# Attention with hashed buckets and two feed-forward layers: q and k arrive feature first, GpSimd splits them, and TensorE no longer transposes them

## What is computed

```
q_bits = (q @ proj > 0);  k_bits = (k @ proj > 0)      # proj is 64 x 6
mask   = (bucket(q_bits)[:, None] == bucket(k_bits)[None, :])
scores = where(mask, 0.125 * q @ k.T, -1e9)
x      = softmax(scores) @ v                            # 16 heads, 768 x 64 each
h = x @ w1_in;  g = where(h > 0, h, exp(min(h, 0)) - 1);  x = g @ w1_out
h = x @ w2_in;  g = s * max(h, 0)**2 + b;                 x = g @ w2_out
```

## Time and profile before

| | |
|---|---|
| median of 3 runs | 829.45 us (828.56 to 829.95) |
| span of the profiled execution, first to last instruction | 824.9 us |
| outside the span, by the runs | 3.7 to 5.1 us |
| TensorE busy | 809.9 us, 98% |
| VectorE, ScalarE, GpSimd busy | 445.3, 364.7, 181.0 us |
| attention | about 0 to 290 us, 17.5 us a head |
| feed-forward | about 290 to 825 us |

### The profile page before, as it was taken

The page is one execution under the profiler, slowest core; times in us unless marked ns, Lnnn a source line. Parts: engine busy times, 40 slices in busy tenths (PEclk is TensorE's granted clock), DMA queues, the critical chain, the costliest instruction groups (busy, mean ns, idle before and its releaser), DMA issues.

```text
span 824.9 us, 12868 instructions
## 1 busy us (share of the span) xinstructions
PE 809.9 (98%) x4252; PEld 697.6 (85%) x4252; DVE 445.3 (54%) x780; ACT 364.7 (44%) x735; POOL 181.0 (22%) x160
## 2 busy tenths in 40 slices
PE   7999999999999999999999999999999999999998
PEld 6799999999999977888888888887888888888886
DVE  6888888888888839533333343335223432243323
ACT  4888888888888831123221222213221222222221
POOL 3243332334322209400000036663000000000000
PEclk9999999999999999999999999999999999999999
DMA  3423243232323013200000012330000100010001
GB/s 97 120 59 94 76 103 91 57 92 74 87 68 88 1 52 125 80 1 0 1 1 1 0 33 94 102 102 26 1 1 0 51 0 0 0 51 0 0 0 51
DMA packets 34359, 38.70 MB, mean 47 GB/s; under 512 B 3168, under 2 KB 25824, under 8 KB 34336
## 3 DMA queue, kind: packets, MB, share of 16 engines
q1 hardware_dynamic: 33744, 38.22, 16.0%
q10 hardware_dynamic: 592, 0.17, 0.1%
HBM read 26.38 MB, written 3.15 MB: 36 GB/s over the span
## 4 chain that ended last, share of the span: by engine, by line
PE 94%; DVE 3%; DMA 1%; ACT 1%; issue 0%; SPq 0%; ACTq 0%; DVEq 0%
PE acc L521 31%; PE h_ps L503 31%; PE pt_ps L466 8%; PE s_ps L457 4%; PE pv_ps L479 4%; PE pv_ps L480 4%; PE s_ps L458 4%; PE prep_ps L434 2%; PE pv_ps L489 2%; PE prep_ps L429 2%; PE prep_ps L439 1%; DVE g_lo L879 1%; PE prep_ps L446 1%; DVE pt_lo L759 1%; DMA qt<-qt 0%
## 5 line engine op out<-in xcount | busy, mean ns | idle before, releaser
L721 ACT ACTIVATE r_sb<-h_ps 128x512 f32<-128x512 f32 x96 | 57.4, 598 | 359.4 <-PE h_ps L503 359.4
L873 DVE TENSOR_SCALAR g_sb<-e_sb,sb_scale 128x512 f32<-128x512 f32 x48 | 26.2, 546 | 158.1 <-ACT e_sb L724 158.1
L759 DVE TENSOR_TENSOR pt_lo<-pt_ps,pt_hi 128x384 fp32r<-128x384 f32 x192 | 103.4, 552 | 13.2 <-ACT pt_hi L627 11.3
L871 DVE SCALAR_TENSOR_TENSOR g_sb<-e_sb,h_ps 128x512 f32<-128x512 f32 x48 | 32.9, 686 | 132.2 <-ACT e_sb L724 132.2
L627 ACT ACTIVATE pt_hi<-pt_ps 128x384 fp32r<-128x384 f32 x192 | 93.4, 494 | 24.5 <-PE pt_ps L466 23.7
L752 DVE TENSOR_REDUCE row_min<-s_ps 128x1 f32<-128x768 f32 x96 | 91.4, 953 | 21.0 <-PE s_ps L458 20.5
L466 PE MATMUL pt_ps<-cst,probs 128*128 128x128 f32 x576 | 95.8, 277 | 1.5 <-DVE pt_lo L759 1.5
L647 ACT ACTIVATE probs<-s_ps,row_min 128x768 f32<-128x768 f32 x96 | 86.7, 904 | 0.9
L879 DVE TENSOR_TENSOR g_lo<-g_sb,g_hi 128x512 fp32r<-128x512 f32 x96 | 80.5, 838 | 3.3
L466 PEld LDWEIGHTS pt_ps<-cst,probs 128*128 128x128 f32 x576 | 68.6, 140 | 12.4 <-issue 6.0
L503 PE MATMUL h_ps<-xt_hi,wa_hi 128*128 (+1 forms) x192 | 75.1, 391 | 0.4 <-DVEq L856 0.4
(11 more groups left out here) (118 smaller groups left out, 1613.2 us busy)
## 6 DMA issues: line engine op xcount, KB each, us to landing
w_raw<-w_in_dram SPq DMA_DIRECT2D x32, 256.0 KB, 2.8
w_raw<-w_out_dram SPq DMA_DIRECT2D x32, 256.0 KB, 2.9
kt<-kt SPq DMA_DIRECT2D x30, 192.0 KB, 2.9
raw_q<-q_dram SPq DMA_DIRECT2D x16, 192.0 KB, 2.4
raw_k<-k_dram SPq DMA_DIRECT2D x16, 192.0 KB, 2.5
raw_v<-v_dram SPq DMA_DIRECT2D x16, 192.0 KB, 2.4
out_dram<-o_sb SPq DMA_DIRECT2D x12, 256.0 KB, 2.1
qt<-qt SPq DMA_DIRECT2D x15, 192.0 KB, 3.7
```

The source lines that it names most:

```text
L759: tt(pt_lo[(k // HT) % 2][where], pt_ps[n][:, 0:HALF].rearrange("p (t c) -> p t c", t=HT), pt_hi[(k // HT) % 2][where].bitcast(F32), ALU.s ...
```

## The change

The host now lays q and k out as `qk[head, feature, {q, k}, token]` and v so that a tile holds consecutive tokens. Every row of SBUF is a feature: rows 0 to 63 and rows 64 to 127 both get all 64 features, of q and of k. The cycles QA to KB are gone with `q_nat`, `k_nat`, `ident_r` and ScalarE's four copies; four cycles stay, in the same units and places. The projections take three matmuls a half (`kt1` holds k hi in both halves, `kt2` k lo over q hi, `qt1` q hi over q lo). GpSimd scales q, rounds and subtracts; SyncE copies q hi twice and k hi no longer.

```diff
-PLAN = ((QA, None, QB), (KA, None, KB), (ZA, None, ZB), (EA, None, None), (EB, None, None), (None, None, None))
+PLAN = ((ZA, None, ZB), (EA, None, None), (EB, None, None), (None, None, None), (None, None, None), (None, None, None))
...
             def load_qk(head):
-                wait(sp, k_split, head)
-                sp.dma_start(raw_q[:].rearrange("p t d -> p (t d)"), row(q_d, head)).then_inc(qk_in, 16)
-                sp.dma_start(raw_k[:].rearrange("p t d -> p (t d)"), row(k_d, head)).then_inc(qk_in, 16)
+                sp.wait_ge(q_split, head)
+                sp.wait_ge(k_split, head)
+                for rows in (slice(0, DH), slice(DH, P)):
+                    sp.dma_start(raw_qk(rows), row(qk, head)).then_inc(qk_in, 16)
+            def load_first():
+                for n, raw, landed in ((0, raw_q, q0_in), (1, raw_k, k0_in)):
+                    for rows in (slice(DH, P), slice(0, DH)):
+                        sp.dma_start(raw[rows, :], qk[0, :, n, :]).then_inc(landed, 16)
...
             def copy_hi(head, par):
-                sp.wait_ge(prep_act, len(BY_ACT) * head + KB + 1)
-                k_hi_rows = kt2[par][DH:P, :].bitcast(F32)
-                sp.dma_start(kt1[par][0:DH, :].bitcast(F32), k_hi_rows).then_inc(hi_copied, 16)
-                sp.dma_start(kt1[par][DH:P, :].bitcast(F32), k_hi_rows).then_inc(hi_copied, 16)
-                sp.dma_start(qt2[par][0:DH, :].bitcast(F32), qt1[par][0:DH, :].bitcast(F32)).then_inc(hi_copied, 16)
+                sp.wait_ge(q_hi, head + 1)
+                q_hi_rows = kt2[par][DH:P, :].bitcast(F32)
+                sp.dma_start(qt1[par][0:DH, :].bitcast(F32), q_hi_rows).then_inc(hi_copied, 16)
+                sp.dma_start(qt2[par][0:DH, :].bitcast(F32), q_hi_rows).then_inc(hi_copied, 16)
+            def step(head, par, v=True, qk=True, copy=True):
+                if v:
+                    load_v(head + 2)
+                if copy:
+                    copy_hi(head + 2, par)
+                if qk:
+                    load_qk(head + 3)
+            def pair(i):
+                step(2 * i, 0)
+                step(2 * i + 1, 1)
+                load_w(0, i, 0, i)
+            load_first()
+            load_v(0)
+            sp.wait_ge(hi_copied, 32)
             load_qk(1)
+            copy_hi(1, 1)
+            load_v(1)
             load_qk(2)
...
             def split_qk(head, par):
...
+                low = slice(DH, P)
+                pool.wait_ge(qk_in, 32 * head)
+                wait(pool, scores_done, TILES * (head - 1))
                 pool.nop(nofuse=True)
+                nc.gpsimd.tensor_scalar(raw_q[:], raw_q[:], -SCALE, 1.0, ALU.mult, ALU.mult).then_inc(q_scaled, 1)
+                nc.gpsimd.tensor_copy(kt1[par][:], raw_k[:]).then_inc(k_hi, 1)
+                pool.wait_ge(q_scaled, head)
+                pool.wait_ge(k_hi, head + 1)
                 pool.nop(nofuse=True)
+                nc.gpsimd.tensor_copy(kt2[par][low, :], raw_q[low, :]).then_inc(q_hi, 1)
+                nc.gpsimd.tensor_tensor(kt2[par][0:DH, :], raw_k[0:DH, :], kt1[par][0:DH, :].bitcast(F32),
+                                        ALU.subtract).then_inc(k_split, 1)
                 pool.wait_ge(q_hi, head + 1)
+                nc.gpsimd.tensor_tensor(qt1[par][low, :], raw_q[low, :], kt2[par][low, :].bitcast(F32),
+                                        ALU.subtract).then_inc(q_split, 1)
+                pool.wait_ge(k_split, head + 1)
+                pool.wait_ge(q_split, head + 1)
...
             def pair(i, more=True):
                 split_v(2 * i + 1, 1)
-                split_qk(2 * i + 3, 1)
-                split_v(2 * i + 2, 0)
                 if more:
-                    split_qk(2 * i + 4, 0)
+                    split_qk(2 * i + 2, 0)
+                    split_v(2 * i + 2, 0)
+                    split_qk(2 * i + 3, 1)
                 split_w(at(wa_hi, i), at(wa_lo, i), i, 0, i + 1)
...
             def prepare(head, par, cycle, bank=prep_ps[:]):
+                if cycle == ZA:
+                    pe.wait_ge(k_split, head + 1)
+                    pe.wait_ge(q_split, head + 1)
+                    pe.wait_ge(hi_copied, 32 * head + 32)
+                if cycle <= ZB:
+                    for j, x in enumerate((kt1, kt2, qt1)):
+                        last = mm(dst, plane(n, j), x[par][:, cols], start=n == 0 and j == 0, stop=n == 1 and j == 2)
...
+            act.wait_ge(q0_in, 32)
+            copy(kt2[0][DH:P, :], raw_q[DH:P, :], -SCALE).then_inc(q_hi, 1)
+            copy(qt1[0][0:DH, :], raw_q[0:DH, :], -SCALE).then_inc(hi_copied, 16)
+            copy(qt2[0][0:DH, :], raw_q[0:DH, :], -SCALE).then_inc(hi_copied, 16)
...
+            nc.vector.scalar_tensor_tensor(qt1[0][low, :], raw_q[low, :], -SCALE, kt2[0][low, :].bitcast(F32),
+                                           ALU.mult, ALU.subtract).then_inc(q_split, 1)
+            dve.wait_ge(k_hi, 1)
+            tt(kt2[0][top, :], raw_k[top, :], kt1[0][top, :].bitcast(F32), ALU.subtract).then_inc(k_split, 1)
```

More of the change, by code:

```diff
@@ L40 @@
 GROUPS = UNITS // HT
-CYCLES = 8
+CYCLES = 4
 TOKENS = BATCH * SEQ
@@ L70, in uses @@
 def uses(k):
[L72 to L74 removed]
+    t, off = k % TILES, k // TILES + 1
+    got = [None if c is None else (off, c) for c in PLAN[t]]
     if k in X_UNIT:
@@ L423, in prepare @@
                 dst = bank[:, 0:HALF]
-                if cycle <= KB:
-                    src, ready = (q_nat, q_split) if cycle <= QB else (k_nat, k_split)
-                    if n == 0:
-                        pe.wait_ge(ready, head + 1)
-                    for r in range(HT):
-                        last = nc.tensor.transpose(bank[:, r * P:(r + 1) * P].bitcast(F32R),
-                                                   src[par][:, n * HT + r, :], ident_r[:])
-                elif cycle <= ZB:
-                    for j, x in enumerate((qt1, qt1, kt2, kt2)):
-                        last = mm(dst, planes[:, n, j, :], x[par][:, cols], start=n == 0 and j == 0, stop=n == 1 and j == 3)
+                if cycle == ZA:
[5 more added lines that the diff above has]
+                        last = mm(dst, plane(n, j), x[par][:, cols], start=n == 0 and j == 0, stop=n == 1 and j == 2)
                 else:
@@ L440, in prepare, with compared @@
                 last.then_inc(prep_pe, 1)
+            def compared(head, half):
+                pe.wait_ge(prep_act, len(BY_ACT) * head + half + 1)
+                pe.wait_ge(prep_dve, len(BY_DVE) * head + half + 2)
             def transpose_x(i, n):
@@ L534, in place @@
                     off, cycle = use
-                    if not (not first if cycle >= XA else main and (more or off < 2)):
-                        return
-                    at = ORDER.index((k, n, use))
-                    last = ORDER[at - 1][2] if at else (1, KB)
-                    if last[1] >= XA:
-                        emptied(i, ORDER[at - 2][2])
-                    if cycle != ZB:
-                        emptied(i, last)
-                    if cycle >= XA:
-                        if cycle == XB:
-                            emptied(i, (0, XA))
-                        transpose_x(i, cycle - XA)
-                    else:
-                        prepare(2 * i + off, off % 2, cycle)
+                    head = 2 * i + off
+                    if cycle >= XA:
+                        if first:
+                            return
+                        half = cycle - XA
+                        if main and (more or half == 0):
+                            compared(2 * i + 1 + half, 1)
+                        else:
+                            pe.wait_ge(xt_lo_done, 2 * i - 2 + half)
+                        transpose_x(i, half)
+                    elif main and (more or off < 2):
+                        if cycle == ZA and k >= TILES:
+                            if first:
+                                compared(head - 1, 1)
+                            else:
+                                pe.wait_ge(xt_lo_done, 2 * i - 1)
+                        elif cycle == ZA and not first:
+                            pe.wait_ge(pt_lo_done, 2 * u - 1)
+                        elif cycle == EB:
+                            compared(head, 0)
+                        prepare(head, off % 2, cycle)
                 turned = (main or k <= HT) and not (first and k < 2 * HT)
@@ L556, in unit @@
                         pe.wait_ge(prep_dve, len(BY_DVE) * head + len(BY_DVE))
-                        pe.wait_ge(hi_copied, 48 * head + 48)
                     scores(u + AHEAD, (k + AHEAD) % UNITS)
-                if first and k == 0:
-                    pe.wait_ge(prep_act, len(BY_ACT) + QB + 1)
                 if main:
```

179 lines of the change are left out of this document (61 added, 118 removed).

## The result

| | before | after |
|---|---|---|
| median | 829.7 us, 4 runs, 828.56 to 830.15 | 838.98 us, 4 runs, 837.3 to 840.92 |
| ratio to before | | 1.0115, 95% interval 1.0096 to 1.0133 |
| span of the profiled execution | 824.9 us | 837.5 us (its own time 839.3) |
| start of the last scores of the attention (timeline of TensorE) | 283.25 us | 296.66 us |
| mean granted clock of TensorE | full | 0.982 |

A forecast was written before the change was run, and what follows sets the result against it. TensorE's issue was taken to bound the kernel, 17.5 us a head. Span 824.9 - 17.6 (savings) + 1.4 (stall) + 4.2 (weight slot) + 2.5 (start) = 815.4, with 4.55 to the median 820.0 us; range 813 to 836.

The forecast's parts named there:

- The 4.55 us: Whole kernel: the median's excess over the profiled span before, added to the forecast span of 815.4 to give 820.0.
- side by side, which I take: GpSimd's split: two 64-row subtractions on different halves overlap, q's starting at 2.65 and done at 4.5 us, not 6.15.
- rival 2: GpSimd's split: 64-row instructions go one after the other, the slot costs 14.4 us instead of 4.2, 830.2; chance 0.18.
- The start: Heads 0 and 1: head 0 loses nothing, ZA of head 1 comes 3.4 late; loss 2.5 us, bounds 0 and 4.
- The 0.35: Projections: two matmuls fewer a head save 0.35 us, 5.3 over 15 heads; also credited before U1 at the start.
- TensorE's savings: Attention units: transposes gone from U4 and U5 save 12.3 us, fewer projection matmuls 5.3, together 17.6.
- rival 3: GpSimd's split: the scaling costs what a two-input instruction does, 1.84 us, 1.0 more; 834.9 us; chance 0.17.
- rival 1: Raw loads: 64-row loads run near 399 GB/s, so the weights' delay is not there; 813.3 us; chance 0.12.
- rival 4: U4 and U5 stay near 2.9 us as VectorE or ScalarE is last; a part would give 824; chance 0.08.
- The deadline at ZA: ZA in U0: the copies of q hi come last, 0.1 us late, a stall of 1.4 us over 14 heads.
- the slot, last on both queues: Weight slot, last in the pair: its split ends late, so ZA of six heads waits 0.7 us more, 4.2 in all.
- the slot's delay is over 2 us: Weight slot: one of the stated signs that the forecast is wrong; the delay forecast was 0.7 us.

The follow-up runs named there:

- e5: Changed kernel with GpSimd splitting a weight slot one head later, behind the next q and k, SyncE's order untouched: 816.97 us, ratio 0.985.
- e3: Changed kernel with eight unread matmuls ahead of ZA in U0 of each second head but the first: 833.24 us, ratio 1.0053.
- e7: Changed kernel with a second raw buffer for q and k, load_qk(1) issued at once: 815.45 us, ratio 0.9824.
- e2: Changed kernel with q and k stored twice by the host, one 128-row load instead of two of 64 rows: 821.54 us, ratio 0.9907.
- e4: Changed kernel with 38 warming matmuls at the start instead of 12: 837.38 us, ratio 1.0093.
- e9: Changed kernel without the addition of 1e-9 to the row sums, the reciprocal reading the sums: 839.29 us, ratio 1.0113.

## Why the prediction was wrong

The spans are compared: forecast 815.4, measured 837.5, 22.1 us apart. The 4.55 us that I added to reach the median was another error, with the other sign: after, the median is 1.5 above the span. Of the 4.55 about 2.0 lie outside the span, and the rest is that the profiled execution was faster than most. Between medians the forecast was off by 19.0 us (820.0 against 838.98).

- **The step that failed: "side by side, which I take".** The rows under the result show the subtractions in series, 1.90 apart, and the split 6.4 us long where 4.5 was taken. That was rival 2's mechanism, at a chance of 0.18. What it costs through the slot: the span of the changed kernel less that of e5 is 837.5 - 815.0 = 22.5 us, of which the clock has 5.7 (e3), so 16.8 are left, nearly all waiting: TensorE's waits at ZA for GpSimd sum to 14.6. Rival 2 had 14.4 for this and I had 4.2. No run makes the subtractions overlap; that they don't is read from the rows, where in all 15 splits both take 1.80 to 1.86. The gap of starts in the earlier trace rows, which leaned to side by side, was no evidence: here too each instruction starts about 0.05 ahead of its predecessor's recorded end or up to 0.16 behind it. The Trainium skill's rule (GPSIMD Engine Reference, Instruction dispatch), that each core goes on by itself, did not show in these rows: two instructions on different halves gained nothing, and 64 rows cost what 128 do (0.83 against 0.82 for the rounding).
- **What no rival had: the clock.** 5.7 us in four spells. I priced a stall as its own length, though the matmuls that follow it were at half rate. That carried the time from rival 2's 830 past the range. Together with the slot's waits this is 22.5 - 4.2 = 18.3 of the 22.1.
- **The start.** Forecast 2.5 us of loss, measured 6.0 at U4 of head 0 (32.33 against 26.37), and 5.8 in e5 (32.14): ZA of head 0 is 1.6 late, where I had nothing, and head 1's split starts at 16.31 after a wait for its load. I credited 0.85 us at full clock, and it ran at the lower one. Some 3.3 of the 22.1, by e5. The 0.35 was also counted twice, here and in the 15 x 0.35 of the savings. e7 shows the cause of half of it: the load that waited for head 0.
- **TensorE's savings** were right in kind and a little too large. e5's pair gives 2.16 us for two heads, forecast 2.26. U5 is 2.41 to 2.42, as the earlier trace rows had it; U4 is 2.63 (2.67 in the changed kernel) and 3.10, not 2.58, with a wait of 0.34 for `pt_lo` in the longer one. I read U4 from one kind of head: the earlier trace rows show a second head's, 2.95, while that of the first heads already took 3.30 before (131.36 to 134.66), so it gave 0.20 us and not 0.37 (the second heads' gave 0.31). To the last scores e5 is 283.25 - 274.39 = 8.9 us ahead, with 5.8 lost at the start: 14.6 saved behind it, against 17.6 - 1.4 = 16.2. That is 1.6 of the 22.1; the remaining 1.0 us has the other sign and lies behind the last scores.
- **What held.** The scaling costs 0.83 us, so rival 3 fell. The 64-row loads run at about 200 GB/s, so rival 1 fell. The Trainium skill's rule (SBUF — State Buffer, Door 1: The DMA port swizzle), that 64 rows reach half of the ports, agrees with the 203 and 199 of the windows. In e2, with one load of 128 rows, the windows from 157 to 160 us show 319 to 356. The units do get shorter, so rival 4 fell. The deadline at ZA is where I put it; in the first heads it costs 0.3, not 0.1, and is set by q's subtraction and not by the copies. And the slot, last on both queues, was the right place to look.

The prediction's own test said that I would be wrong if "the slot's delay is over 2 us". It is 3.0.

What stays open: why one long stall leaves the clock up. Here it was the first, of 2.63 us. In e4 and in e9, which have the same five stalls, four were again followed by the lower clock, and the one that was not was another: the last in e4 (2.41 us, clock 1.00 from 257.5 to 261 us), the second in e9 (2.32 us, 1.00 from 148.3 to 151.8). So neither its length nor its place among the five decides it alone. The other half of the loss at the start was not taken apart, and why U4 of first heads takes 3.10 was not tried either.

## What to carry to other kernels

In a queue that is served in order, an item that is due late must not stand ahead of one that is due early: moving a load by one step, or its consumer by one head, was worth 21 us of 839, more than the whole change could save. Before work moves to an engine with slack, write down when each of its products is due and add up its queue in series; take overlap within an engine only from a row that shows it. And a stall of TensorE like these, of 2.3 to 2.5 us, should be priced with what the clock takes behind it (here 5.7 us over four, 1.4 a stall).

## What was not expected of the hardware

- GpSimd: 64x768 costs 0.83 us rounded, as 128x768 does (0.82), and 1.83 subtracted, as estimated for 128 rows from the earlier trace rows; instructions on disjoint halves did not overlap in any of the 15 splits.
- VectorE: a TENSOR_SCALAR within SBUF on 128x3 took up to 2.33 us, until a running GpSimd instruction ended; TENSOR_REDUCE on PSUM and RECIPROCAL beside such instructions kept 0.95 and 0.18.
- TensorE: four waits of 2.3 to 2.5 us were each followed by matmuls at 0.32 instead of 0.175 apart, one of 2.63 was not. Eight matmuls in the wait kept the full rate. The clock column can be wrong near the start of a trace: in e5 it reads 1.00 from 10 to 24 us, while the scores from 14.87 to 16.79 start 0.32 apart, the lower rate. The distance between starts is the surer reading.
- DMA: two loads of 64 rows and 384 KB, issued 0.6 us apart, were both there 6.1 us after the first issue; one of 128 rows and 768 KB took 4.6 (median of 15: 4.3).
